# Router scores of the first 1536 tokens computed between the last attention rounds instead of behind them

## The chip, the cores and the metric

One Trainium2 chip, one of its cores. The metric is device time in microseconds (us), the median of several executions; lower is better. Engines are called PE (TensorE), DVE (VectorE), ACT (ScalarE), POOL (GpSimd) and SP (SyncE, which issues most DMAs).

## The reference

Three layers follow each other. Batch 4, 8 heads, 576 positions, head size 64, so 2304 tokens of width 512.

```python
scores = q @ k.T / 8                       # masked: 4 heads local (32 back), 4 heads strided (every 32nd)
attn = exp(scores - max) / (sum + 1e-9)
x = (attn @ v)  -> [2304, 512]
skip_score = x @ w_skip                    # > 0: the token goes to an expert, else it is passed on
logits = x[do] @ w_gate                    # 8 experts, the largest logit chooses; gate = its softmax value
x[do] += gate * (relu(x[do] @ w1[e]) @ w2[e])
h = x @ w_in;  g = h>=1: h, h<=-1: 0, else (h+1)^2/4
out = g @ w_out
```

What the change touches is the product of x with `w_gate` and `w_skip` together, nine scores for a token.

## The kernel before, in words

**Attention.** It is cut into 20 steps (`STEPS`, five for each of four batches of 576 tokens). A round of PE (L915 to L918, and the unrolled epilogue at L919 to L925) does for three different steps: `turn` (L868, four 128x128 transposes of the probabilities), `scores` (not in the epilogue) and `values` (L876, many small products on 64x64 tiles of the array). DVE takes maxima and sums, POOL scales the probabilities (L447, semaphore `normed`), ACT does the exponentials, copies the turned probabilities out of PSUM (L528, `turn_copied`) and places the result of `values` in the tile XT (L537, L543, L546, `x_placed`). `values(n)` waits for `turn_copied` of its own step and for `x_placed` of the step before, since all steps use the same PSUM pair `out_b` (banks 4 and 5).

The epilogue serves steps 16 to 19: the loop is over `range(STEPS, STEPS + LAST)` with LAST = 4, so s = 20, 21, 22, 23, and a pass does `turn(s - 3)` and `values(s - 4)`. The first three passes have both, the fourth has `values(19)` alone. Between them stand products with zeros that nobody reads (`busy`, L829, bf16, 128x512, into bank 3): 1, 0, 1, 0 of them after the four turns (`BUSY_TURNED`) and 4, 0, 2, 2 after the four values (`BUSY_VALUED`).

**Scores of the router.** Behind the epilogue PE waits for all 20 steps to be placed and runs `logits` (L934). The weights `wgs` are 32 columns wide (9 used), and four strips of 512 tokens are put on four 32-column tiles of the array (`out[32*j : 32*(j+1)]`), accumulated over the four 128-blocks of the width (c). That is 16 products of 512 tokens in bank 4, then 8 of 128 tokens (two strips) in bank 5. The scores stand with the score down the partitions, so they are copied (`lgT`, DVE L687, ACT L558), transposed back (PE L946, L949) and copied to `lg` with the token down the partitions (DVE L689, L691).

**Routing.** DVE does a chain of small operations on `lg` (L692 to L740), in which each waits for the one before. Three other engines take part. ACT computes the exponentials (L564), but only behind its copy of row tile 4 (`EXP_AT`). PE computes the ranks of the tokens (L956, L957) behind its row tile 7 (`RANKS_BEHIND`). DVE then ends in `slot_of` (L717), the place of each token in the order sorted by expert.

**Rows.** Meanwhile PE turns XT to rows, 18 tiles of 128 tokens (`rows`, L928, four transposes each, into banks 0 to 3 in turn), and ACT copies each out (L561). PE does `rows(0)` and `rows(1)` ahead of the transposes of the scores and the other 16 behind them.

**Scatter.** When `slot_of` is there, POOL issues 18 indirect DMAs (L456), one after the other, which write the rows to DRAM in sorted order. PE waits for the last eight of them (`late_out`) and runs more products that nobody reads meanwhile (L965). SP waits for all 18, then loads the first windows back (`xfirst`, L368), PE turns them (L970), and the experts begin (L1000, L1010). Behind the experts come the two dense products (L1043, L1056), which take more than half of the time.

**Queues.** SP issues the first three expert weight loads of 2 MB each (L352, L355) when `values(19)` is done.

Of the kernel before, what the change touches and what calls it, by code (L numbers as in the profile page):

```python
# [9 lines left out]
F32 = mybir.dt.float32  # L10
# [8 lines left out]
P = 128  # L19
B, H, S, HD = 4, 8, 576, 64  # L20
STRIDE = 32
PHASE = S // STRIDE
D, E, FE, FF = H * HD, 8, 1024, 2048
N = B * S
NT = N // P
DC, FEC, FFC = D // P, FE // P, FF // P
# [45 lines left out]
TB = len(TILES_OF)  # L72
STEPS = B * TB
# [2 lines left out]
RANKS_BEHIND = 7  # L76
START_BUSY = 10
BUSY_FIRST = [6, 6, 0, 0, 0]
BUSY_TURNED = [1, 0, 1, 0]
BUSY_VALUED = [4, 0, 2, 2]  # L80
BUSY_FROM, BUSY_SCATTER, BUSY_LOAD = 10, 4, 8
SLOTS = TB
LAG, LAST = 3, 4
# [13 lines left out]
REST = N - FULL * G  # L97
EXTRA = (N - 1) // WIN
LGW = 32


MASKS = 5
# [8 lines left out]
def program(nc, qT, kT, vl, vs, wg, w1, w2, win, wout, cst, out):  # L111
    with ExitStack() as ctx:
        def sem(name):
            return ctx.enter_context(nc.semaphore(name))
# [4 lines left out]
        def at(name, shape, dt, offset=None):  # L119
            size = int(np.prod(shape[1:])) * (2 if dt == BF16 else 4)  # L120
            size = (size + 63) // 64 * 64
            where = top[0] if offset is None else offset
            t = nc.alloc_sbuf_tensor_at(name, list(shape), dt, offset=where)
            if offset is None:
                top[0] += size
            return t, where, where + size


        XT, _, _ = at("XT", [P, DC, XCOLS], F32)

        WE1, w_at, w_end = at("WE1", [P, 2, DC, FE], F32)
        WE2, _, w_end = at("WE2", [P, 2, FEC, D], F32)
        o = w_at
        q_loc, _, o = at("q_loc", [P, 2, S], F32, o)
        k_loc, _, o = at("k_loc", [P, 2, S], F32, o)
        v_loc, _, o = at("v_loc", [P, LOC, 4 * HD], F32, o)
        q_str, _, o = at("q_str", [P, 2, S], F32, o)
        k_str, _, o = at("k_str", [P, 2, S], F32, o)
        v_str, _, o = at("v_str", [P, STRIP_PAIRS - 1, 4 * HD], F32, o)
        v_rest, _, o = at("v_rest", [P, 3, 4 * HD], F32, o)  # L140
        assert o <= w_end
        WOH, _, o = at("WOH", [P, FFC, D], F32R, w_at)
        WOL, _, o = at("WOL", [P, FFC, D], F32R, o)
        assert o <= w_end

        WIH, r_at, _ = at("WIH", [P, DC, FF], F32R)
        WIL, _, r_end = at("WIL", [P, DC, FF], F32R)
        xrow, _, o = at("xrow", [P, NT, ROW], F32, r_at)
        prob, p_at, o = at("prob", [P, SLOTS, 512], F32, o)
        probT, _, o = at("probT", [P, 3, 512], F32, o)  # L150
        assert o <= r_end
        gateT, _, o = at("gateT", [E, XCOLS], F32, p_at)
        assert o <= r_end

        hid, h_at, _ = at("hid", [P, 2, FEC, WIN], F32)
        xw, _, _ = at("xw", [P, BUFS, DC, WIN], F32)
        gb, _, _ = at("gb", [P, 2, WIN], F32)
# [13 lines left out]
        cl, _, _ = at("cl", [P, G], F32)  # L171
# [19 lines left out]

        NE9, NE8 = NT * (E + 1), NT * E
        o = h_at
        lgT, _, o = at("lgT", [P, 512 + P], F32, o)
        lg, _, o = at("lg", [P, NT, E + 1], F32, o)
        top8, _, o = at("top8", [P, NT], F32, o)
        dif, _, o = at("dif", [P, NT, E], F32, o)
# [27 lines left out]
        idle_b = bank[3]  # L225
        probT_b = bank[2]
        row_b, logit_b, gate_b = bank[0:4], bank[6], bank[7]
        lgT_b, lgT_rest_b = bank[4], bank[5]
        hid_b, y_b = bank[0:2], bank[2:6]
        first_b, sort_b = bank[2:6], bank[2:6]  # L230
        h2_b, fin_b = bank[6:8], bank[0:4]
# [14 lines left out]
        summed, guarded, inverted, normed, turned, turn_copied = sem("summed"), sem("guarded"), sem("inverted"), sem("normed"), sem("turned"), sem("turn_copied")  # L246
        pv_done, x_placed = sem("pv_done"), sem("x_placed")
        rows_ready, rows_copied, logits_ready = sem("rows_ready"), sem("rows_copied"), sem("logits_ready")
        lgT_ready, lgT_main, lgT_rest, lg_main = sem("lgT_ready"), sem("lgT_main"), sem("lgT_rest"), sem("lg_main")
        route, dif_ready, oh_ready, exp_ready, ranks_ready, slots_ready, aux_ready, starts_ready = sem("route"), sem("dif_ready"), sem("oh_ready"), sem("exp_ready"), sem("ranks_ready"), sem("slots_ready"), sem("aux_ready"), sem("starts_ready")  # L250
        scattered, pads_out = sem("scattered"), sem("pads_out")
        late_out = [sem(f"late_out{t}") for t in range(BUSY_FROM, NT)]
# [267 lines left out]
        def _(act):  # L520
# [33 lines left out]
                if 0 <= s - LAST:  # L554
                    place(s - LAST)

            act.wait_ge(lgT_ready, 2)
            act.copy(lgT[0:2 * LGW, 512:512 + P], lgT_rest_b[0:2 * LGW, 0:P]).then_inc(lgT_rest, 1)  # L558
            for t in range(NT):
                act.wait_ge(rows_ready, t + 1)  # L560
                act.copy(xrow[:, t, 0:D], row_b[t % 4][:, :]).then_inc(rows_copied, 1)  # L561
# [77 lines left out]
        def _(dve):  # L639
# [34 lines left out]
            def link(ins):  # L674
                ins.then_inc(route, 1)
                done[0] += 1
                dve.wait_ge(route, done[0])
# [6 lines left out]
            dve.tensor_copy(xrow[:, :, AUX + E], con[:, C_TOK:C_TOK + NT]).then_inc(aux_ready, 1)  # L684
            link(dve.memset(ones[:, :], 1.0))
            dve.wait_ge(lgT_ready, 1)
            dve.tensor_copy(lgT[:, 0:512], lgT_b[:, :]).then_inc(lgT_main, 1)  # L687
            dve.wait_ge(logits_ready, 2)
            dve.tensor_copy(lg[:, 0:16, :].rearrange("p (j q) e -> p q j e", q=4), logit_b[:, :].rearrange("p (q j e) -> p q j e", q=4, j=4)[:, :, :, 0:E + 1]).then_inc(lg_main, 1)  # L689
            dve.wait_ge(lg_main, 1)  # L690
            link(dve.tensor_copy(lg[:, 16:NT, :], gate_b[:, 0:2 * LGW].rearrange("p (j e) -> p j e", j=2)[:, :, 0:E + 1]))  # L691
            link(dve.tensor_reduce(top8[:, :], lg[:, :, 0:E], AX_X, ALU.max))  # L692
            link(dve.tensor_tensor(dif[:, :, :], lg[:, :, 0:E], tiles(top8[:, :]), ALU.subtract))
            dve.sem_inc(dif_ready, 1)
# [131 lines left out]
        def _(pe):  # L826


            def busy(products, out=None):  # L829

                for _ in range(products):
                    pe.matmul(idle_b[:, :] if out is None else out, warm[:, 0:P], warm[:, :], start=True, stop=True)
# [66 lines left out]
            def round_of(scoring, turning, valuing):  # L899

                if turning:
                    turn(*turning[:2])
                scores(*scoring)
                if valuing:
                    values(*valuing)
# [7 lines left out]
            with pe.Fori(0, LOOPS) as b:  # L913
                for k in range(FIRST, FIRST + TB):
                    round_of(*((TB * b + k - lag, (k - lag) % TB, b + (k - lag) // TB) for lag in (0, LAG, LAST)))  # L915
            for s in range(STEPS, STEPS + LAST):
                if step(s - LAG):
                    turn(*step(s - LAG)[:2])  # L918
                busy(BUSY_TURNED[s - STEPS])  # L919
                values(*step(s - LAST))  # L920
                busy(BUSY_VALUED[s - STEPS])


            pe.wait_ge(wg_in, 16)
            pe.wait_ge(con_in, 16)  # L925
            pe.wait_ge(x_placed, STEPS)
            def rows(t):
# [3 lines left out]
                    last = pe.transpose(row_b[t % 4][:, P * c:P * (c + 1)], XT[:, c, P * t:P * (t + 1)], ident)  # L931
                last.then_inc(rows_ready, 1)

            def logits(out, width, first, groups):  # L934
                for c in range(DC):
                    for j in range(groups):
                        last = pe.matmul(out[LGW * j:LGW * (j + 1), 0:width], wgs[:, c, :], XT[:, c, first + width * j:first + width * (j + 1)], start=(c == 0), stop=(c == DC - 1), skip_group_check=True)  # L937
                last.then_inc(lgT_ready, 1)

            logits(lgT_b, 512, 0, 4)  # L940
            logits(lgT_rest_b, P, 2048, 2)
            for t in range(2):
                rows(t)
            pe.wait_ge(lgT_main, 1)
            for q in range(4):
                last = pe.transpose(logit_b[:, P * q:P * (q + 1)], lgT[:, P * q:P * (q + 1)], ident)  # L946
            last.then_inc(logits_ready, 1)
            pe.wait_ge(lgT_rest, 1)
            pe.transpose(gate_b[:, 0:2 * LGW], lgT[0:2 * LGW, 512:512 + P], ident[0:2 * LGW, 0:2 * LGW]).then_inc(logits_ready, 1)  # L949
            for t in range(2, NT):  # L950
                rows(t)
                if t == RANKS_BEHIND:
# [185 lines left out]
```

## Time and profile before

| what | us |
|---|---|
| runs of the kernel | 687.99, 693.40, 691.78; median 691.78 |
| the profiled execution, its own time | 691.78 |
| its span, first to last instruction | 690.0 |
| attention, up to the end of the last `values` | 0 to 80.1 |
| router scores, routing, scatter, first windows | 80.1 to 125.6 |
| experts | 125.6 to 283.7 |
| dense products and output | 283.7 to 690 |

The profiled execution's own time is 1.8 us more than its span. Over the whole span PE is busy 94%, DVE 46%, ACT 27%, POOL 18%, and the mean granted clock of TensorE is 0.974 of full speed. Each of the stages in the table begins with what the one before it leaves.

### The profile page before, as it was taken

What the parts mean: (1) busy time and instruction counts of PE and PEld (TensorE: products, weight loads), DVE (VectorE), ACT (ScalarE), POOL (GpSimd) and SP (SyncE); (2) the same over time, 40 slices, a digit from 0 to 9 for tenths busy, and PEclk for the clock granted to TensorE, in tenths of its full rate; (3) what the DMA queues carried; (4) which work ended last, traced back from release to release, by engine and by line L of the source; (5) the groups of instructions that cost most, each with busy time, mean ns of one, the idle gap of its engine ahead of it and who ended that gap; (6) DMA issues with size and microseconds to landing.
All of it is one profiled execution on the core that took longest, in us unless ns stands there. A gap on an engine that the chain in (4) does not pass through costs nothing.

```text
span 690.0 us, 12493 instructions
## 1 busy us (share of the span) xinstructions
PE 648.0 (94%) x5190; PEld 553.9 (80%) x5195; DVE 314.8 (46%) x570; ACT 187.9 (27%) x361; POOL 126.9 (18%) x135
## 2 busy tenths in 40 slices
PE   7888856899999999899999999999999999999995
PEld 3767642899999999788888888888888888888994
DVE  4766250141122121675446644456545565545652
ACT  2545450141111111222224222233222332223331
POOL 1323145002222224882000200002000020000201
PEclk9999986999999999999999999999999999999998
DMA  8676495964777775330000100001000010000100
GB/s 285 225 257 226 166 359 198 352 228 167 262 253 255 257 258 178 94 106 16 1 0 1 62 0 1 0 1 61 0 0 0 0 61 0 0 0 0 62 1 30
DMA packets 39477, 76.34 MB, mean 111 GB/s; under 512 B 3079, under 2 KB 17844, under 8 KB 38916
## 3 DMA queue, kind: packets, MB, share of 16 engines
q1 hardware_dynamic: 36556, 66.26, 28.1%
q0 software_dynamic: 2880, 9.52, 3.6%
q8 instruction: 28, 0.46, 0.3%
q14 instruction: 13, 0.11, 0.1%
HBM read 65.83 MB, written 9.94 MB: 110 GB/s over the span
## 4 chain that ended last, share of the span: by engine, by line
PE 81%; DMA 9%; POOL 3%; DVE 2%; issue 1%; SPq 1%; ACT 1%; DVEq 0%
PE pair L1043 28%; PE pair L1056 16%; PE bank L1056 13%; PE pair L1000 9%; DMA WE<-w 4%; PE out_pair L1010 4%; PE bank L1010 4%; DMA k_str<-kT 2%; POOL x_sorted L456 2%; PE out_pair L895 2%; PE pair L853 2%; DMA k_loc<-kT 1%; PE bank L873 1%; DMA xfirst<-x_sorted 1%; PE out_pair L937 1%
## 5 line engine op out<-in xcount | busy, mean ns | idle before, releaser
L1043 PE MATMUL pair<-yh,WIH 128*128 128x512 f32 (+1 forms) x320 | 116.7, 371 | 0.2 <-ACT yh L596 0.2
L1043 PE MATMUL pair<-yh,WIL 128*128 128x512 f32 (+1 forms) x320 | 116.5, 370 | 0.0
L620 ACT ACTIVATE cl<-cl,half 128x512 f32<-128x512 f32 (+1 forms) x80 | 54.5, 681 | 186.9 <-DVE cl L808 185.5
L816 DVE TENSOR_TENSOR gl<-gr,gh 128x512 fp32r<-128x512 f32 (+1 forms) x80 | 54.1, 677 | 73.6 <-ACT gh L629 72.5
L808 DVE TENSOR_SCALAR cl<-pair 128x512 f32<-128x512 f32 (+1 forms) x80 | 50.9, 637 | 73.0 <-PE pair L1043 73.0
L515 POOL DMA_INDIRECT out<-XT,tok x18 | 18.6, 1031 | 351.6 <-DVE XT L796 347.6
L1043 PE MATMUL pair<-yl,WIH 128*128 128x512 f32 (+1 forms) x320 | 79.7, 369 | 1.7 <-DVE yl L787 1.7
L1000 PE MATMUL pair<-xw,WE 128*128 128x168 f32 x512 | 76.2, 311 | 0.2
L1000 PEld LDWEIGHTS pair<-xw,WE 128*128 128x128 f32 x512 | 74.8, 193 | 0.8 <-DMA WE<-w 0.7
L1043 PEld LDWEIGHTS pair<-yh,WIH 128*128 128x128 f32 x320 | 60.7, 190 | 11.3 <-ACT yh L596 0.6
L629 ACT CAST gh<-gr 128x512 fp32r<-128x512 f32 (+1 forms) x80 | 46.3, 579 | 86.0 <-PE bank L1056 61.0
L1043 PEld LDWEIGHTS pair<-yh,WIL 128*128 128x128 f32 x320 | 60.9, 190 | 10.7
L1043 PEld LDWEIGHTS pair<-yl,WIH 128*128 128x128 f32 x320 | 57.0, 189 | 12.7 <-DVE yl L787 2.8
L814 DVE TENSOR_TENSOR gr<-gr,cl 128x512 f32<-128x512 f32 (+1 forms) x80 | 52.7, 659 | 22.3 <-ACT cl L620 22.0
L1056 PE MATMUL pair<-WOH,gh 128*128 128x512 f32 x160 | 62.5, 391 | 0.0
L1056 PE MATMUL pair<-WOL,gh 128*128 128x512 f32 x160 | 62.4, 390 | 0.0
L1056 PE MATMUL pair<-WOH,gl 128*128 128x512 f32 x160 | 62.3, 389 | 0.0
L811 DVE TENSOR_SCALAR gr<-pair 128x512 f32<-128x512 f32 (+1 forms) x80 | 50.1, 627 | 0.0
L577 ACT ACTIVATE hid<-pair 128x168 f32<-128x168 f32 x64 | 19.9, 310 | 110.2 <-PE pair L1000 110.2
L1056 PE MATMUL bank<-WOH,gh 128*128 128x512 f32 x128 | 49.8, 389 | 0.0
L1056 PE MATMUL bank<-WOL,gh 128*128 128x512 f32 x128 | 49.8, 389 | 0.0
L1056 PE MATMUL bank<-WOH,gl 128*128 128x512 f32 x128 | 49.8, 389 | 0.0
(144 smaller groups left out, 814.4 us busy)
## 6 DMA issues: line engine op xcount, KB each, us to landing
WE<-w SPq DMA_DIRECT2D x16, 2048.0 KB, 12.3
xrow<-x_sorted SPq DMA_DIRECT2D x6, 781.5 KB, 9.1
v_loc<-vl SPq DMA_DIRECT2D x4, 1024.0 KB, 7.8
raw_in<-win SPq DMA_DIRECT2D x16, 256.0 KB, 9.5
raw_out<-wout SPq DMA_DIRECT2D x16, 256.0 KB, 2.6
q_loc<-qT SPq DMA_DIRECT2D x4, 576.0 KB, 6.1
k_loc<-kT SPq DMA_DIRECT2D x4, 576.0 KB, 8.1
v_str<-vs SPq DMA_DIRECT2D x8, 256.0 KB, 4.2
```

Source lines behind the costliest of these rows:

```text
L515: pool.indirect_dma_start(out, bass.IndirectOffsetOnAxis(tok[:, GT * g + t:GT * g + t + 1], 0), rows_of(g, t), None).then_inc(out_done if ...
L577: act.activation(hid[:, par, f, :], hid_b[f % 2][:, 0:WIN], ACT.Relu).then_inc(h_done, 1)
L620: act.activation(cl[:, 0:n], cl[:, 0:n], ACT.Square, bias=half[:, :], scale=0.5).then_inc(squared, 1)
L629: act.copy(gh[:, f % 2, 0:n], gr[:, 0:n]).then_inc(g_high, 1)
L808: dve.tensor_scalar(cl[:, 0:n], h2_b[f % 2][:, 0:n], -1.0, 1.0, ALU.max, ALU.min).then_inc(clamped, 1)
L811: dve.tensor_scalar(gr[:, 0:n], h2_b[f % 2][:, 0:n], 1.0, -1.0, ALU.max, ALU.add).then_inc(over, 1)
L814: dve.tensor_tensor(gr[:, 0:n], gr[:, 0:n], cl[:, 0:n], ALU.add).then_inc(g_ready, 1)
L816: dve.tensor_tensor(gl[:, f % 2, 0:n], gr[:, 0:n], gh[:, f % 2, 0:n].bitcast(F32), ALU.subtract).then_inc(g_low, 1)
L1000: last = pe.matmul(hid_b[f % 2][:, 0:WIN], WE1[:, par, c, P * f:P * (f + 1)], xw[:, buf, c, :], start=(c == 0), stop=(c == DC - 1))
L1010: last = pe.matmul(y_b[c][:, 0:WIN], WE2[:, par, f, P * c:P * (c + 1)], hid[:, par, f, :], start=(f == 0), stop=(f == FEC - 1))
L1043: last = pe.matmul(h2_b[f % 2][:, 0:tokens], w[:, c, P * f:P * (f + 1)], x[:, c, 0:tokens], start=(k == 0), stop=(k == 3 * DC - 1))
L1056: last = pe.matmul(fin_b[t][:, :], x[:, f % 2, P * t:P * (t + 1)], w[:, f, :], start=(f == 0 and k == 0), stop=(f == FFC - 1 and k == 2))
```

## The change

The scores are cut anew: three strips of 512 tokens (tokens 0 to 1535, `EARLY`) and three strips of 256 tokens (tokens 1536 to 2303, `LATE`).

```diff
-BUSY_TURNED = [1, 0, 1, 0]
-BUSY_VALUED = [4, 0, 2, 2]
+STRIPS, EARLY, LATE = 3, 512, 256
+LG_EARLY = STRIPS * EARLY // P
-        lgT_b, lgT_rest_b = bank[4], bank[5]
+        lgT_b, lgT_rest_b = bank[3], bank[4]
...
-            act.wait_ge(lgT_ready, 2)
-            act.copy(lgT[0:2 * LGW, 512:512 + P], lgT_rest_b[0:2 * LGW, 0:P]).then_inc(lgT_rest, 1)
...
             dve.wait_ge(lgT_ready, 1)
-            dve.tensor_copy(lgT[:, 0:512], lgT_b[:, :]).then_inc(lgT_main, 1)
-            dve.wait_ge(logits_ready, 2)
-            dve.tensor_copy(lg[:, 0:16, :].rearrange("p (j q) e -> p q j e", q=4), logit_b[:, :].rearrange("p (q j e) -> p q j e", q=4, j=4)[:, :, :, 0:E + 1]).then_inc(lg_main, 1)
-            dve.wait_ge(lg_main, 1)
-            link(dve.tensor_copy(lg[:, 16:NT, :], gate_b[:, 0:2 * LGW].rearrange("p (j e) -> p j e", j=2)[:, :, 0:E + 1]))
+            dve.tensor_copy(lgT[0:STRIPS * LGW, 0:EARLY], lgT_b[0:STRIPS * LGW, :]).then_inc(lgT_main, 1)
+            dve.wait_ge(lgT_ready, 2)
+            dve.tensor_copy(lgT[0:STRIPS * LGW, EARLY:EARLY + LATE], lgT_rest_b[0:STRIPS * LGW, 0:LATE]).then_inc(lgT_rest, 1)
+            for k, (first, last, turned_b) in enumerate(((0, LG_EARLY, logit_b), (LG_EARLY, NT, gate_b))):
+                q = (last - first) // STRIPS
+                dve.wait_ge(logits_ready, k + 1)
+                link(dve.tensor_copy(lg[:, first:last, :].rearrange("p (j q) e -> p q j e", q=q),
+                                     turned_b[:, 0:(last - first) * LGW].rearrange("p (q j e) -> p q j e", q=q, j=STRIPS)[:, :, :, 0:E + 1]))
...
+            def logits(out, width, first, c):
+                for j in range(STRIPS):
+                    last = pe.matmul(out[LGW * j:LGW * (j + 1), 0:width], wgs[:, c, :], XT[:, c, first + width * j:first + width * (j + 1)], start=(c == 0), stop=(c == DC - 1), skip_group_check=True)
+                if c == DC - 1:
+                    last.then_inc(lgT_ready, 1)
             for s in range(STEPS, STEPS + LAST):
                 if step(s - LAG):
                     turn(*step(s - LAG)[:2])
-                busy(BUSY_TURNED[s - STEPS])
+                if s == STEPS + 2:
+                    logits(lgT_b, EARLY, 0, 1)
                 values(*step(s - LAST))
-                busy(BUSY_VALUED[s - STEPS])
-            pe.wait_ge(wg_in, 16)
+                if s == STEPS:
+                    pe.wait_ge(wg_in, 16)
+                    pe.wait_ge(x_placed, TB * (B - 1))
+                    logits(lgT_b, EARLY, 0, 0)
+                elif s >= STEPS + 2:
+                    logits(lgT_b, EARLY, 0, s - STEPS)
             pe.wait_ge(con_in, 16)
             pe.wait_ge(x_placed, STEPS)
...
-            logits(lgT_b, 512, 0, 4)
-            logits(lgT_rest_b, P, 2048, 2)
+            for c in range(DC):
+                logits(lgT_rest_b, LATE, STRIPS * EARLY, c)
+            for k, (at_, width, turned_b, signal) in enumerate(((0, EARLY, logit_b, lgT_main), (EARLY, LATE, gate_b, lgT_rest))):
+                pe.wait_ge(signal, 1)
+                for q in range(width // P):
+                    last = pe.transpose(turned_b[:, STRIPS * LGW * q:STRIPS * LGW * (q + 1)], lgT[0:STRIPS * LGW, at_ + P * q:at_ + P * (q + 1)], ident[0:STRIPS * LGW, 0:STRIPS * LGW])
+                last.then_inc(logits_ready, 1)
             for t in range(2):
                 rows(t)
-            pe.wait_ge(lgT_main, 1)
-            for q in range(4):
-                last = pe.transpose(logit_b[:, P * q:P * (q + 1)], lgT[:, P * q:P * (q + 1)], ident)
-            last.then_inc(logits_ready, 1)
-            pe.wait_ge(lgT_rest, 1)
-            pe.transpose(gate_b[:, 0:2 * LGW], lgT[0:2 * LGW, 512:512 + P], ident[0:2 * LGW, 0:2 * LGW]).then_inc(logits_ready, 1)
```

So a slice, three products of 512 tokens for one c, stands behind `values(16)` (c = 0), ahead of `values(18)` (c = 1), behind `values(18)` (c = 2) and behind `values(19)` (c = 3). All `busy` products of the epilogue go. The transposes of the scores stand ahead of `rows(0)` and `rows(1)`, and the copy of the second part of `lgT` goes from ACT to DVE.

## Rows read from the trace of the kernel before

**Rows 1.** The profile page, its part 4: the chain that ended last, by engine.
```profile
PE 81%; DMA 9%; POOL 3%; DVE 2%; issue 1%; SPq 1%; ACT 1%; DVEq 0%
```

**Rows 2.** Timeline of PE, 66 to 104 us; columns: start us, length us, engine, line, operation
```profile
71.57 0.73 PE L895 MATMUL out_pair<-probT,v_str 64*64 64x54 f32 x32 [0.44 <-ACT XT L537]
72.23 1.04 PE L832 MATMUL bank<-warm 128*128 128x512 bf16 x4
73.46 0.66 PE L873 MATMUL bank<-con,prob 128*128 128x128 f32 x4 [0.19 <-POOL prob L447]
74.04 1.05 PE L895 MATMUL out_pair<-probT,v_rest 64*64 64x54 f32 x48
75.02 0.65 PE L873 MATMUL bank<-con,prob 128*128 128x128 f32 x4
76.09 1.74 PE L895 MATMUL out_pair<-probT,v_loc 64*64 64x32 f32 x64 [0.42 <-ACT XT L543]
...
78.59 1.46 PE L895 MATMUL out_pair<-probT,v_loc 64*64 64x32 f32 x64 [0.23 <-ACT XT L546]
...
80.83 4.50 PE L937 MATMUL out_pair<-XT,wgs 128*32 128x512 f32 x48 [0.24 <-ACT XT L546]
85.26 1.09 PE L931 MATMUL pair<-con,XT 128*128 128x128 f32 x8
86.19 0.60 PE L946 MATMUL pair<-con,lgT 128*128 128x128 f32 x4
...
90.04 0.54 PE L956 MATMUL pair<-oh,con 128*128 128x162 f32 x2 [0.28 <-DVEq L702]
```

**Rows 3.** Timeline of DVE, 70 to 128 us
```profile
84.59 0.69 DVE L687 COPY lgT<-out_pair 128x512 f32<-128x512 f32 x1 [10.72 <-PE out_pair L937]
...
87.58 0.30 DVE L692 TENSOR_REDUCE top<-lg 128x18 f32<-128x144 f32 x1
...
90.08 0.30 DVE L705 TENSOR_REDUCE gate<-ex 128x18 f32<-128x144 f32 x1 [0.15 <-DVE oh L701]
...
91.15 0.32 DVE L711 COPY tot<-pair 128x162 f32<-128x162 f32 x1
...
93.59 0.18 DVE L717 CAST slot_of<-posf 128x18 uint32<-128x18 f32 x1
```

**Rows 4.** Timeline of POOL, 66 to 128 us: first and last of the 18 scatters
```profile
94.06 1.14 POOL L456 DMA_INDIRECT x_sorted<-xrow,slot_of  x1 [13.64 <-ACT xrow L561]
...
115.74 0.96 POOL L456 DMA_INDIRECT x_sorted<-xrow,slot_of  x1 [0.30 <-issue]
```

**Rows 5.** Timeline of PE's weight loads (PEld), 66 to 128 us
```profile
81.25 0.15 PEld L937 LDWEIGHTS out_pair<-XT,wgs 128*32 128x32 f32 x4 [0.28 <-issue]
81.68 0.16 PEld L937 LDWEIGHTS out_pair<-XT,wgs 128*32 128x32 f32 x4 [0.27 <-issue]
...
84.26 0.80 PEld L937 LDWEIGHTS out_pair<-XT,wgs 128*32 128x32 f32 x14 [0.28 <-issue]
```

**Rows 6.** Timeline of ACT, 66 to 128 us
```profile
80.09 0.58 ACT L546 COPY XT<-out_pair 128x512 f32<-128x512 f32 x1 [1.65 <-PE out_pair L895]
...
85.95 1.07 ACT L561 COPY xrow<-pair 128x512 f32<-128x512 f32 x2 [0.33 <-PE pair L931]
...
89.05 0.35 ACT L564 ACTIVATE ex<-dif 128x144 f32<-128x144 f32 x1
...
95.15 1.18 ACT L561 COPY xrow<-pair 128x512 f32<-128x512 f32 x2
```

**Rows 7.** Timeline of PE, 105 to 190 us: products of the first two experts
```profile
125.61 11.01 PE L1000 MATMUL pair<-xw,WE 128*128 128x168 f32 x64
...
146.27 9.29 PE L1000 MATMUL pair<-xw,WE 128*128 128x168 f32 x64
```

**Rows 8.** Busy time by 2 us: PE, PEld, DVE, ACT, POOL, PEclk, DMA share, GB/s
```profile
122.00:124.00 2.00, 0.32 (x3) 0.32 (x4) 0.00 (x0) 0.00 (x0) 0.00 (x0) 1.00 0.73 188
...
126.00:128.00 2.00, 2.00 (x8) 2.00 (x8) 0.02 (x1) 0.01 (x1) 0.00 (x0) 0.50 1.00 382
```

More of the change, by code:

```diff
@@ L99 @@
 LGW = 32
+STRIPS, EARLY, LATE = 3, 512, 256
+LG_EARLY = STRIPS * EARLY // P
+assert STRIPS * (EARLY + LATE) == N and STRIPS * EARLY <= (B - 1) * S
 MASKS = 5
@@ L193, in program @@
         o = h_at
-        lgT, _, o = at("lgT", [P, 512 + P], F32, o)
+        lgT, _, o = at("lgT", [P, EARLY + LATE], F32, o)
         lg, _, o = at("lg", [P, NT, E + 1], F32, o)
@@ L248, in program @@
         rows_ready, rows_copied, logits_ready = sem("rows_ready"), sem("rows_copied"), sem("logits_ready")
-        lgT_ready, lgT_main, lgT_rest, lg_main = sem("lgT_ready"), sem("lgT_main"), sem("lgT_rest"), sem("lg_main")
+        lgT_ready, lgT_main, lgT_rest = sem("lgT_ready"), sem("lgT_main"), sem("lgT_rest")
         route, dif_ready, oh_ready, exp_ready, ranks_ready, slots_ready, aux_ready, starts_ready = sem("route"), sem("dif_ready"), sem("oh_ready"), sem("exp_ready"), sem("ranks_ready"), sem("slots_ready"), sem("aux_ready"), sem("starts_ready")
@@ L932, in rows @@
                 last.then_inc(rows_ready, 1)
[L934 to L938, printed above, removed]
-            logits(lgT_b, 512, 0, 4)
-            logits(lgT_rest_b, P, 2048, 2)
+            for c in range(DC):
[5 more added lines that the diff above has]
+                last.then_inc(logits_ready, 1)
             for t in range(2):
                 rows(t)
-            pe.wait_ge(lgT_main, 1)
-            for q in range(4):
-                last = pe.transpose(logit_b[:, P * q:P * (q + 1)], lgT[:, P * q:P * (q + 1)], ident)
-            last.then_inc(logits_ready, 1)
-            pe.wait_ge(lgT_rest, 1)
-            pe.transpose(gate_b[:, 0:2 * LGW], lgT[0:2 * LGW, 512:512 + P], ident[0:2 * LGW, 0:2 * LGW]).then_inc(logits_ready, 1)
             for t in range(2, NT):
```

## The prediction, made before the changed kernel was run

> **What bounds the kernel now.** I read the chain that ended last first. PE holds 81% of it [rows 1], so over the whole span the kernel is bound by products. That says nothing of the stretch that the change touches, so I went on to the timelines from 70 to 128 us, one engine at a time.
>
> There the chain goes in single file: last attention steps, router scores, transposes, DVE's routing chain, scatter, experts. The reader should see three things. First, the last `values` start on an ACT copy: at 76.09 and 78.59 PE had been idle for 0.42 and 0.23 us and was released by XT L543 and L546 [rows 2], although products that nobody reads stand in the gaps. Second, behind the placement of step 19 (ACT, 80.09 plus 0.58 [rows 6]) PE needs 4.50 us for the scores, and the routing chain reads `lg` at 87.58 only [rows 2, 3]. Third, POOL starts its 18 scatters at 94.06, 0.3 us after `slot_of` (93.59 plus 0.18), and issues them at one per (115.74 - 94.06) / 17 = 1.275 us, whatever the others do [rows 3, 4]. The rows are copied faster than that (18 from 85.95 to 96.33 us [rows 6]), so the scatter begins with `slot_of`, and the experts begin a fixed time behind the scatter. What moves `slot_of` moves the end.
>
> **The change part by part.**
>
> *What a slice costs.* The four 32-column tiles work beside each other: four weight loads come per 0.43 us (81.25 to 81.68 [rows 5]), and each 512-token product has two such records, so one c of four strips takes 2 x 0.43 = 0.86 us. Three strips on three tiles should take the same 0.86 us, since each tile has its own strip to stream. Bounds: 0.64 us, if the time goes by the number of products (6 x 0.107), and 6 x 0.43 = 2.6 us, if the strips ran one after another. I take 0.86, since the rows show exactly this form with one tile more. Between array layouts (128x128 turns, 64x64 values) the rows leave little: four turns at 73.46, at 0.11 us each, are followed by values at 74.04, so 0.14 us at most. I add 0.10 us ahead of each slice and 0.14 behind.
>
> The Trainium skill (TensorEngine Tiling (Array Packing), Key Properties) says that changing the tiling mode drains TensorE. That speaks against slicing, because each slice brings layout changes that the scores in one piece do not have. By the rows' 0.14 us the drain is already in my sum; the page gives no figure of its own.
>
> *c = 0, behind `values(16)`.* It takes the place of four products (72.23, 1.04 us) ahead of the turn at 73.46, which waits for POOL (0.19 us idle [rows 2]). Values end at about 72.25; 0.10 + 0.86 + 0.14 gives 73.35. It costs 0. The cover is POOL's scaling, with 0.1 us left. The waits on `wg_in` and on 15 placed steps are long met: values of step 16 themselves waited for 16.
>
> *c = 1, ahead of `values(18)`.* The turns at 75.02 issue until 75.46 (4 x 0.11). With the slice values(18) start at 75.46 + 1.10 = 76.56 in place of 76.09: **+0.47 us**. Queued behind it on PE is all that follows, and ACT's placement waits for it.
>
> *c = 2, behind `values(18)`.* From the start of values(18) to that of values(19) it is 78.59 - 76.09 = 2.50 us now, of which about 1.6 are the values' own issue. With the slice it is 1.6 + 1.10 = 2.7: **+0.2 us**. So values(19) start at 79.26, its placement at 80.76, ending at 81.34.
>
> *c = 3 and the late strips.* Values(19) issue until 80.66; the slice runs to 81.62, behind the placement, so the wait for step 20 placed costs nothing. The late part is 4 c of 2 records of 256 tokens: 8 x 0.214 = 1.71 us, to 83.33. Before, the scores ended at 80.83 + 4.50 = 85.33. The 128-token part took 0.80 us for 14 of 16 loads [rows 5]; 24 loads at that rate take 1.4 us and stay under 1.71.
>
> *The way to `lg`.* DVE's copy of the first part (0.69 us [rows 3]) runs beside the late strips. Its four transposes take 0.44 us, to 83.87. The copy of the second part, 256 wide, begins at 83.5; between the 162-wide copy (0.32) and the 512-wide one (0.69 [rows 3]) I take 0.42, so 83.95; two transposes end at 84.35; the second copy to `lg` ends at 84.70. (Before, `rows(0)` and `rows(1)` stood ahead: 86.19 - 85.26 = 0.93 us [rows 2].) The routing chain begins at 84.70 in place of 87.58: **-2.88 us**.
>
> *What is late next.* The chain does not keep all of that. Rows now begin at 84.25, 1.0 us earlier than 85.26, and not 2.9. ACT's first copy goes from 85.95 to about 84.94; five copies at 0.53 us (1.07 for two [rows 6]) and the exponential of 0.35 us end at 87.75 or so (between 87.5 and 88.1). DVE, with everything else shifted, would want it at 90.08 - 2.88 = 87.20. So the reduction L705 starts near 87.80: 0.6 us are given back, and the shift is **-2.28 us**. The ranks: eight row tiles at 0.435 us from 84.25 end at 87.73, and 0.82 us more for the ranks is 88.55, against DVE's need at 91.15 - 2.28 = 88.87 [rows 2, 3]. This wait has 0.3 us left.
>
> *Behind it.* `slot_of` comes 2.3 us earlier, so the scatter starts at 91.8. The expert weights are asked for by the end of values(19), 0.67 us later than before, and are needed at 125.6 less 2.3, so this costs 0. They share the DMA engines with the early scatters; only the last scatters are waited for, and those are issued at POOL's own pace. All later DMAs hang on events that move along. The copy moved from ACT to DVE has 0.42 us, already in the sum.
>
> The sum: the profiled execution took 691.78 us, span 690.0 and 1.8 around it, and is the median of the runs. 691.78 - 2.28 = 689.5.
>
> **The rivals.**
>
> *The clock's low spells shift.* In the first expert the granted clock stands at 0.50 of full speed (1.2 in place of 2.4 GHz) at 126 to 128 us, after PE had done only 0.32 us of work at 122 to 124 [rows 8]. That expert's 64 products take 11.01 us where the next one's take 9.29: a spell costs 1.7 us [rows 7]. The spell comes late after the idle time, so another moment of arrival may avoid it or add one: 687.8 or 691.2. For it: the spread of the runs, 5.4 us. Against: PE's pattern ahead of the experts is the same, only earlier. The lost filling products are not a way to a new spell, I think: their time is taken by slices.
>
> *ACT keeps up.* If exponential and ranks do not hold DVE, all 2.88 us come through: 688.9. It needs copies at 0.45 us, faster than any row.
>
> *ACT's row copies bound the scatter.* The row of the first scatter names the ACT copy as releaser [rows 4]. Then only the 1.0 us of the rows count: 690.8. Against: the first scatter needs one copied tile, and that was there at 86.5.
>
> *Slower: strips in single file.* If three strips in a slice do not overlap because both records of one product must finish ahead of the next product, a slice takes up to 2.6 us. With x for a slice, c = 1, 2, 3 and the late part (two slices' worth) put 5 x on the path, and the gain of 2.28 is gone at x = 0.86 + 2.28 / 5 = 1.3 us. At 2.6 it is 5 x 1.7 more, and c = 0 overruns its cover by 1.5: 691.8 - 2.3 + 8.5 + 1.5 = 699.5. Against: four strips in the same order overlap fully now [rows 5].
>
> *It does not do what it says* (nothing moves, because the wait for POOL or ACT in the last rounds sets all): excluded by the 4.50 us, which have no such wait in them.
>
> **How the numbers follow.** Forecast 689.5 with chance 0.60; a low spell less 0.12; one more 0.12; all 2.88 us 0.06; bound by row copies 0.05; strips in single file 0.03; something outside this stretch by more than 1%, 0.02. A measurement of this kernel can tell about 1% (7 us) from no change. All cases but the last two lie within it: same 0.95, faster 0.02, slower 0.03. The range takes in the clock cases at 687.8 and 691.2 and 1 us more each side for the spread of the runs, whose median moves by about that: 686.8 to 692.3.
>
> **What would show it right or wrong.** Right: 24 + 24 records of 512 and 256 tokens in place of 32 and 16; values(18) and (19) start 0.47 and 0.67 us later; reduction L692 at 84.7; DVE idle for about 0.6 us ahead of the reduction of the gates, released by ACT; first scatter near 91.8, last near 113.5; experts from 123.3; equal lengths behind. Wrong: a slice of more than 1.1 us; the turn behind c = 0 later than 73.5; a new fall of the clock between 72 and 90 us; a wait of DVE for the ranks; an expert stage that starts earlier but lasts longer.

## The result, and the profile after

The changed kernel took 685.86 us (median of 20 runs, 681.68 to 689.11), the kernel before 689.29 (20 runs, 686.29 to 694.03): ratio 0.994, 95% interval 0.9922 to 0.9958, that is 4.1 us less (2.9 to 5.4). The ratio is one of means (685.86 and 689.84); the medians lie 3.4 us apart. The forecast was 689.5 with a range from 686.8, so the time lies 0.9 us below the range. Two later copies of the changed kernel gave 0.9965 (0.9937 to 0.9993) and 0.9955 (0.9928 to 0.9982).

The profiled execution took 683.28 us, its span is 681.5, 8.5 less than before. Most of that does not lie where the change acts. I cut both spans at the turns of step 18 (the second last four turns of probabilities), the first scatter, the first expert's first product, and the first turn of sorted rows behind that expert:

| stretch, us | before | after | difference |
|---|---|---|---|
| start to turns of step 18 (of the change only the slice behind `values(16)` lies here) | 73.46 | 70.83 | -2.63 |
| turns of step 18 to first scatter (the change) | 20.60 | 17.86 | -2.74 |
| first scatter to first expert | 31.55 | 30.28 | -1.27 |
| first expert's 64 products | 10.84 | 9.23 | -1.61 |
| the rest of the span | 553.55 | 553.30 | -0.25 |

Timeline of PE of the changed kernel, 70 to 100 us, which answers to [rows 2] (columns as there; L876 are the turns, L898 the values, L921 the slices and late strips, L945 the rows):

```profile
69.59 1.06 PE L921 MATMUL bank<-XT,wgs 128*32 128x512 f32 x6
70.83 0.66 PE L876 MATMUL bank<-con,prob 128*128 128x128 f32 x4 [0.18 <-POOL prob L449]
...
72.39 0.66 PE L876 MATMUL bank<-con,prob 128*128 128x128 f32 x4
72.98 1.06 PE L921 MATMUL bank<-XT,wgs 128*32 128x512 f32 x6
73.97 1.46 PE L898 MATMUL out_pair<-probT,v_loc 64*64 64x32 f32 x64
75.35 1.06 PE L921 MATMUL bank<-XT,wgs 128*32 128x512 f32 x6
76.34 1.45 PE L898 MATMUL out_pair<-probT,v_loc 64*64 64x32 f32 x64
77.73 1.06 PE L921 MATMUL bank<-XT,wgs 128*32 128x512 f32 x6
78.61 1.90 PE L921 MATMUL out_pair<-XT,wgs 128*32 128x256 f32 x24
80.44 0.99 PE L953 MATMUL pair<-con,lgT 96*128 96x96 f32 x6
81.27 1.04 PE L945 MATMUL pair<-con,XT 128*128 128x128 f32 x8
```

The turns at 70.83 still wait for POOL, so the slice ahead of them was free. From 72.39 on PE has no idle time left between these rows, where [rows 2] has 0.42, 0.23 and 0.24 us. (Of the 0.42 us a part was filled: the trace of before has records of six of the ten filling products. The trace of e12, a run of the same attention code that is described below, has all ten, and 0.21 us idle there.) A slice is 72.98 to 73.97, 0.99 us. Two times 0.43 us are the products, as in [rows 5], and 0.13 us are left behind them; ahead of the slice it is 0.15 us (72.39 to 72.98, less 4 x 0.11 for the turns). The Trainium skill (TensorEngine Tiling (Array Packing), Key Properties) says that changing the tiling mode drains TensorE. The trace agrees in so far as these 0.13 and 0.15 us lie at the changes of layout; no run here shows that a drain is what fills them.

Timeline of DVE of the changed kernel, 70 to 128 us, for [rows 3]:

```profile
81.78 0.30 DVE L695 TENSOR_REDUCE top<-lg 128x18 f32<-128x144 f32 x1
...
84.70 0.30 DVE L708 TENSOR_REDUCE gate<-ex 128x18 f32<-128x144 f32 x1 [0.57 <-ACT ex L564]
...
88.21 0.18 DVE L720 CAST slot_of<-posf 128x18 uint32<-128x18 f32 x1
```

Timeline of POOL, the same stretch, first and last scatter, for [rows 4]:

```profile
88.69 1.14 POOL L458 DMA_INDIRECT x_sorted<-xrow,slot_of  x1 [10.52 <-ACT xrow L561]
...
110.42 0.96 POOL L458 DMA_INDIRECT x_sorted<-xrow,slot_of  x1 [0.30 <-issue]
```

The reduction of the largest score is L695 here and L692 in the kernel before; below I call it L692 in both. The new wait is in the second line of DVE: it stands for 0.57 us until the exponential is done, where before it waited only 0.15 us behind its own work [rows 3].

Behind the scatter, for [rows 7], timeline of PE, 98 to 190 us:

```profile
116.55 0.97 PE L977 MATMUL bank<-con,xfirst 128*128 128x128 f32 x8
118.02 1.03 PE L977 MATMUL out_pair<-con,xfirst 128*128 128x128 f32 x8 [0.49 <-DMA xfirst<-x_sorted]
118.97 9.39 PE L1007 MATMUL pair<-xw,WE 128*128 128x168 f32 x64
```

The idle time ahead of the first expert is short here, and it runs at full clock. Whether that is the change's was the question for the experiments.

### The profile page after: what moved, and what is told of

Read it like the earlier page. It is cut to its first block, busy times and chain, and to the rows that moved or that the text cites. A ratio compares the mean times of both kernels' runs of the same rounds, so it can differ in the third digit from the quotient of the medians.

```text
span 681.5 us, 12481 instructions
## 1 busy us (share of the span) xinstructions
PE 641.6 (94%) x5185; PEld 548.7 (81%) x5186; DVE 316.6 (46%) x571; ACT 188.0 (28%) x360; POOL 126.7 (19%) x135
## 4 chain that ended last, share of the span: by engine, by line
PE 84%; DMA 6%; POOL 3%; DVE 2%; issue 1%; ACT 1%; SPq 1%; DVEq 0%
PE pair L1050 29%; PE pair L1063 16%; PE bank L1063 13%; PE pair L1007 10%; PE out_pair L1017 5%; PE bank L1017 5%; DMA k_loc<-kT 3%; POOL x_sorted L458 2%; DMA WE<-w 2%; PE out_pair L898 2%; PE pair L856 2%; ACT xrow L561 1%; PE bank L876 1%; DVE yl L790 1%; PE bank L991 1%
## 5 line engine op out<-in xcount | busy, mean ns | idle before, releaser
L1007 PE MATMUL pair<-xw,WE 128*128 128x168 f32 x512 | 74.5, 306 | 0.2 <-DMA WE<-w 0.2
L1007 PEld LDWEIGHTS pair<-xw,WE 128*128 128x128 f32 x512 | 73.2, 190 | 0.5 <-DMA WE<-w 0.5
## 6 DMA issues: line engine op xcount, KB each, us to landing
xrow<-x_sorted SPq DMA_DIRECT2D x6, 781.5 KB, 10.2
```

Of the source, the lines that this page charges most:

```text
L1007: last = pe.matmul(hid_b[f % 2][:, 0:WIN], WE1[:, par, c, P * f:P * (f + 1)], xw[:, buf, c, :], start=(c == 0), stop=(c == DC - 1))
```

## The experiments

All stretches are those of the table, in us of one profiled execution; median and ratio are those of 12 runs (six for e9). "xf" is last scatter to the first turns of xfirst.

| run | edit | start to turns of 18 | to first scatter | scatter to expert | xf | first expert | rest | median us | ratio (95%) |
|---|---|---|---|---|---|---|---|---|---|
| e0 | before | 72.66 | 20.35 | 31.44 | 7.84 | 10.90 | 550.85 | 688.62 | 0.9996 (0.997 to 1.0022) |
| e2 | new cut, not moved | 73.68 | 20.83 | 31.47 | 7.56 | 10.46 | 551.86 | 688.96 | 0.9996 (0.9961 to 1.0031) |
| e3 | turns of scores first | 70.24 | 19.87 | 33.07 | 8.16 | 11.00 | 553.12 | 688.42 | 1.0009 (0.998 to 1.0037) |
| e6 | before, no fill | 75.94 | 23.14 | 30.91 | 6.13 | 9.23 | 552.98 | 688.76 | 0.9992 (0.9968 to 1.0016) |
| e10 | before, no fill | 72.89 | 23.17 | 31.38 | 5.81 | 10.16 | 552.90 | 692.33, one run | |
| e12 | before, padded | 70.84 | 20.69 | 30.94 | 6.17 | 10.90 | 550.93 | 688.48 | 0.9999 (0.9971 to 1.0028) |
| e1 | after | 74.73 | 17.86 | 31.05 | 6.17 | 10.90 | 552.96 | 685.79 | 0.9965 (0.9937 to 0.9993) |
| e14 | after | 74.46 | 17.85 | 31.17 | 5.82 | 10.90 | 553.12 | 686.53 | 0.9955 (0.9928 to 0.9982) |
| e7 | after, padded | 71.32 | 17.85 | 31.84 | 7.44 | 11.54 | 553.55 | 687.34 | 0.9957 (0.9935 to 0.9979) |
| e13 | after, padded | 73.29 | 17.86 | 30.99 | 6.68 | 10.66 | 553.00 | 685.78 | 0.9953 (0.9928 to 0.9979) |
| e8 | slice c = 0 late | 73.35 | 20.25 | 30.39 | 5.91 | 9.23 | 553.28 | 687.53 | 0.9965 (0.9945 to 0.9985) |
| e4 | exponential early | 73.31 | 17.60 | 31.05 | 6.22 | 10.47 | 553.37 | 687.61, one run | |
| e5 | and ranks early | 74.97 | 17.44 | 30.89 | 6.02 | 10.90 | 551.00 | 685.18 | 0.9949 (0.9923 to 0.9975) |
| e11 | as e5 | 71.03 | 17.43 | 30.90 | 5.88 | 10.90 | 550.34 | 684.62 | 0.9947 (0.9927 to 0.9966) |
| e9 | e5 and four fills | 70.36 | 17.45 | 31.45 | 5.96 | 9.23 | 553.01 | 683.10 | 0.992 (0.9895 to 0.9946) |
| e15 | e9, padded | 70.85 | 17.43 | 31.20 | 6.25 | 9.22 | 549.80 | 683.75 | 0.9926 (0.9898 to 0.9953) |

**The changed kernel again (e1), and the kernel before again (e0).**

> The changed kernel once more, for a second profile. Stretches are measured from the start of the second last pair of turns that wait for POOL, the turns of step 18 (before 73.46 us, after 70.83 us). Theory A (the change gives a fixed 2.75 us between the turns of step 18 and the first scatter; the remaining difference of the two profiled spans is spread from run to run): turns of step 18 to first scatter 17.9 us again, but start to the turns of step 18 anywhere in 70 to 74 us, first scatter to first expert 30.2 to 31.6, first expert's 64 products 9.3 or 11.0. Theory B (the change itself also makes the transfers and the clock behind the scatter better): first scatter to first expert 30.3 again and first expert 9.3 again. Time 0.994 to 0.996 of before.

> The kernel before once more, for a second profile. Theory C: behind the scatter the kernels differ because an instruction fetch (one packet of the queue of kind instruction) falls beside the loads of the first windows (xfirst) in the kernel before, at 120 us, and not in the changed one, whose PE program is nine products shorter up to there. Then here again: a fetch between the first xfirst load and the first turns of xfirst; last scatter to the first of these turns 7.5 to 8.2 us (after: 6.0 to 6.2), first scatter to first expert 31.5 or more. Theory A (spread from run to run): values like those of the changed kernel, 6.1 and 30.3 to 31.1, are as likely.

The stretch of the change repeats to 0.01 us (17.86), the others do not: e1 starts its turns 3.9 us later than the first profile and has a first expert of 10.90 us, for the same program. So theory A (spread from run to run) holds for the attention and the first expert, whose 2.63 and 1.61 us are spread. The granted clock goes with the spread. In the five profiles in which it stood at 1.00 up to the turns of step 18 (after, e3, e7, e9, e12) these come at 70.2 to 71.3 us, in the thirteen others, with a mean of 0.93 to 0.98, at 70.9 to 75.9. The first expert takes 9.2 us in the five profiles in which the clock stands at 1.00 all through it (after, e6, e8, e9, e15) and 10.2 to 11.5 in the thirteen in which it is at 0.50 for a part. And the rest of the span is 552.9 to 553.6 us in the twelve profiles in which the clock falls to 0.50 between 281 and 296 us, and 549.8 to 551.9 in the six in which it does not (e0, e2, e5, e11, e12, e15). Kernels with and without the change are on either side each time but one (no kernel with the filling products of before has the 9.2), so the spread is not tied to the change as far as is shown. e1's ratio, 0.9965, is just above the expected 0.994 to 0.996. xf repeats in each kernel (6.13, 6.17 against 7.94, 7.84), which A did not say.

**The new cut without the move (e2).**

```diff
+                busy(BUSY_TURNED[s - STEPS])
                 values(*step(s - LAST))
+                busy(BUSY_VALUED[s - STEPS])
-                if s == STEPS + 2:
-                    logits(lgT_b, EARLY, 0, 1)
-                if s == STEPS:
...
-                    pe.wait_ge(x_placed, TB * (B - 1))
-                    logits(lgT_b, EARLY, 0, 0)
-                elif s >= STEPS + 2:
-                    logits(lgT_b, EARLY, 0, s - STEPS)
...
+            for c in range(DC):
+                logits(lgT_b, EARLY, 0, c)
```

> Three strips of 512 and three of 256 tokens and the turns of the scores ahead of the rows, but all of it behind the attention, with the filling products back in the epilogue. If the move between the last rounds is what brings the gain: turns of step 18 to first scatter 20.8 us (before 20.6, after 17.9), time within 0.1% of before. Rival (the new cut and the new order of the turns bring it): below 19.5 us.

20.83 us, and a ratio of 0.9996: the cut and the new order of the turns alone bring nothing (before and e0 have 20.60 and 20.35). The move, with the filling products that it replaces, brings 20.83 - 17.86 = 2.97.

**Only the turns of the scores ahead of the rows (e3).**

> The kernel before with one edit: the turns of the scores ahead of rows 0 and 1. The reduction L692 comes 0.9 us earlier against the turns of step 18. If the exponential behind ACT's copy of row tile 4 holds DVE, 0.4 us of it are given back: turns of step 18 to first scatter 20.1 us. If it does not: 19.7.

Against e0, whose values take the same 1.46 us, the reduction L692 comes 0.79 us earlier and the scatter 0.48. DVE waits 0.47 us for the exponential. So 0.3 us, two fifths of what the order of the turns gives, are lost to the same wait. As time the 0.48 us do not show (ratio 1.0009).

**The exponential and the ranks (e5, e4).** `EXP_AT = 4` to 1, and in e5 `RANKS_BEHIND = 7` to 6.

> The changed kernel with the exponential behind ACT's copy 1 instead of 4 and the ranks behind row tile 6 instead of 7. If the wait of 0.57 us ahead of the reduction of the gates is the exponential's place in ACT's queue: the wait goes, turns of step 18 to first scatter 17.3 us (after 17.9), time about 0.9992 of after. If something else holds DVE there, 17.9.

> The changed kernel with only the exponential moved, behind copy 1. The wait of 0.57 us for it goes; then the ranks, behind row tile 7, come 0.2 to 0.3 us too late for DVE: turns of step 18 to first scatter 17.6 to 17.7 us, between 17.86 (changed kernel) and 17.44 (both moved).

Timeline of DVE, e4, 82 to 94 us:

```profile
86.76 0.30 DVE L708 TENSOR_REDUCE gate<-ex 128x18 f32<-128x144 f32 x1 [0.15 <-DVE oh L704]
...
87.60 0.31 DVE L711 TENSOR_TENSOR xrow<-oh,gate 128x144 f32<-128x144 f32 x1
87.99 0.33 DVE L714 COPY tot<-pair 128x162 f32<-128x162 f32 x1
```

The wait for the exponential is gone. L714 begins 0.39 us after L711 where it is 0.22 in the changed kernel (85.55 to 85.77): the ranks are late next, by 0.17 us. With both moved the stretch is 17.44, 0.42 less (expected 17.3). Both steps were as expected in the trace; the time of e5 and e11 (0.9949 and 0.9947) can't be told from that of the changed kernel, 0.994 to 0.9965.

**The filling products and the slice behind step 16 (e6, e10, e8).** e6 and e10 set `BUSY_TURNED` and `BUSY_VALUED` of the kernel before to zero. e8 is the changed kernel with the slices c = 0 ahead of values(18), 1 behind them, 2 and 3 behind values(19), and none behind step 16.

> The kernel before without the ten products that nobody reads in the epilogue of the attention, nothing else. Turns of step 18 to first scatter as before, 20.3 to 20.6 us. Theory C: the PE program is ten products shorter, so the fetch moves into the first expert, and last scatter to first turns of xfirst falls to 6.1 us, first scatter to first expert to 30.3 to 31.1; time about 0.9985 of before. Theory A: 7.5 to 8.2 and 31.5 as in the kernel before. If the filling products hold the clock up, the granted clock falls between 72 and 90 us and the stretch gets over 1 us longer.

> The kernel before without its ten filling products, a second profile. Last scatter to first turns of xfirst 6.1 us again, whatever the clock does. The fall of the clock at 81 to 87 us that its first profile showed may come again (turns of step 18 to first scatter 23.1 us) or not (20.3): it depends on when the idle gaps fall.

> The changed kernel with one slice fewer behind values of step 16 and one more behind values of step 19. If the slice behind step 16 is free and one behind step 19 costs its whole 0.86 us: turns of step 18 to the reduction L692 11.8 us (after 10.95), to first scatter 18.7 (after 17.9). If slices cost nothing because something else ends last: 17.9.

Both profiles without fill have the same 2.8 us more (23.14, 23.17 against e0's 20.35). Busy time by 2 us of e6 (columns: PE, PEld, DVE, ACT, POOL, granted clock, DMA share, GB/s):

```profile
78.00:80.00 2.00, 1.58 (x66) 1.37 (x64) 0.00 (x0) 0.87 (x4) 0.00 (x0) 1.00 0.00 0
80.00:82.00 2.00, 1.22 (x40) 1.22 (x40) 0.00 (x0) 0.58 (x1) 0.00 (x0) 0.73 0.03 8
82.00:84.00 2.00, 1.22 (x39) 1.12 (x36) 0.00 (x0) 0.59 (x1) 0.23 (x1) 0.50 0.00 0
```

Timeline of PE of e6, 70 to 98 us:

```profile
75.94 0.66 PE L873 MATMUL bank<-con,prob 128*128 128x128 f32 x4 [1.17 <-POOL prob L447]
...
80.81 2.40 PE L895 MATMUL out_pair<-probT,v_loc 64*64 64x32 f32 x64 [0.78 <-ACT XT L546]
83.99 6.34 PE L937 MATMUL out_pair<-XT,wgs 128*32 128x512 f32 x48 [0.78 <-ACT XT L546]
```

With the gaps left open (1.17 us ahead of the turns of step 18, 0.42 ahead of values(18), 0.78 ahead of values(19) and of the scores), the clock goes from 2.4 to 1.2 GHz, and the scores take 6.34 us where they took 4.50 [rows 2]. Which of the gaps it takes is not shown. Nor does the loss show in the runs: e6 has 0.9992 (0.9968 to 1.0016) of before, so at most 1.1 us more, and its profiled execution, 693.96 us, was one of its slowest. The fall may be a matter of single executions, or be made up for behind the scatter. e8 missed its expectation, 20.25 in place of 18.7, by a fall of the clock too. Timeline of PE of e8, 70 to 98 us:

```profile
73.35 0.63 PE L876 MATMUL bank<-con,prob 128*128 128x128 f32 x4 [1.37 <-POOL prob L449]
...
76.17 1.93 PE L921 MATMUL bank<-XT,wgs 128*32 128x512 f32 x6
```

Busy time of e8 by 2 us:

```profile
72.00:74.00 2.00, 0.65 (x6) 0.51 (x8) 1.50 (x5) 0.94 (x3) 1.60 (x2) 1.00 0.04 12
74.00:76.00 2.00, 2.00 (x52) 1.79 (x52) 0.00 (x0) 1.35 (x4) 0.48 (x1) 0.64 0.00 0
76.00:78.00 2.00, 2.00 (x8) 0.20 (x6) 0.00 (x0) 0.63 (x2) 0.00 (x0) 0.51 0.00 0
78.00:80.00 2.00, 2.00 (x73) 1.50 (x70) 0.00 (x0) 0.47 (x1) 0.00 (x0) 1.00 0.04 8
```

PE stands idle for 1.37 us ahead of the turns, the clock falls, and values(18) begin 1.54 us later (4.68 after the turns of step 18, against 3.14). L692 comes at 13.35 after them: 10.95, plus 1.54, plus 0.86 for the slice that now lies on the path. So the slice behind step 16 is free, and in this profile its absence also let the clock fall. The time does not show these 2.4 us: e8 has 687.53 us, and e7, the changed kernel with padding measured beside it, 687.34. The Trainium skill (TensorE: Matmul & The Clock Gate, What's actually happening) says that the throttled state is the default and activity releases it. The trace agrees: the clock is at 0.51 at 76 to 78 us, behind the idle time, and back at 1.00 at 78 to 80, with PE busy from 74 us on.

**Where the instruction fetch falls (e7, e12, e13, e14).** The trace has two queues of kind instruction, which I read as the engines' instruction fetches. One, q14, puts a packet of 8 KB some 2.9 to 4.0 us behind the first xfirst load in every profile. The other, q8, with packets of 16 KB, is the one that moves, and "the fetch" is its packet. In the kernel before, it comes at 120.8 us, between the first xfirst load (118.65) and the first turns of xfirst (123.68); in the changed kernel, whose PE program is nine products shorter up to there, it comes at 121.6 us, in the first expert (118.97 to 128.2). e7 and e13 put nine products into PE's idle time behind the last row tile of the changed kernel, e12 puts 36 there in the kernel before:

```diff
             pe.wait_ge(slots_ready, 1)
+            for _ in range(9):
+                pe.matmul(bank[0][:, :], ident_b[:, :], mask_b[:, 0, :].unsqueeze(1).to_broadcast([P, 8, KEYS]), start=True, stop=True)
```

> The changed kernel with nine products that nobody reads put on PE behind its last row tile, where it then sits idle for 15 us: the PE program is as long again as before up to the first windows. Turns of step 18 to first scatter 17.9 us as in the changed kernel. Theory C: a fetch beside the loads of xfirst again, last scatter to first turns of xfirst 7.5 to 8.2 us, first scatter to first expert 31.5. Theory A: 6.1 and 30.3 to 31.1.

> The kernel before with 36 products that nobody reads behind PE's last row tile, where PE then sits idle: they lengthen the PE program, so that the instruction fetch comes earlier, ahead of the loads of xfirst. Turns of step 18 to first scatter 20.3 to 20.6 us as before. Theory C: last scatter to first turns of xfirst falls from 7.8 to 6.0 us and first scatter to first expert from 31.5 to 30.3 to 31.1; time 0.9985 of before. Rival (what helps is the changed scores, not where the fetch falls): 7.8 and 31.5.

> The changed kernel with nine products of padding once more, beside the changed kernel itself. Theory C: last scatter to first turns of xfirst 7.4 to 8.2 us, first scatter to first expert 31.4 or more, time about 1 us over the changed kernel. Rival: no difference.

> The changed kernel a third time, as the partner of the padded one. Turns of step 18 to first scatter 17.86 us, last scatter to first turns of xfirst 6.0 to 6.2, first scatter to first expert 30.3 to 31.1; time 0.9945 to 0.995 of before if 2.5 to 2.75 us of the new order and about 1 us of the fetch add up.

The fetch lies between first load and first turns in before, e0, e2, e3, e7, e13: xf is 7.4 to 8.2 us in five of the six, 6.68 in e13. In the twelve others it lies elsewhere, and xf is 5.8 to 6.25. e12 moves it by padding alone (to 108.6 us) and xf falls from 7.84 to 6.17; e6 moves it the other way (to 132.4 us) with the same result. So when the first window is ready goes with the place of the fetch. It is worth less behind that, since PE also needs the second window: scatter to first expert has a mean of 31.73 us over those six and 30.97 over the twelve. A third of this 0.8 us is e3 alone (33.07); the medians are 31.51 and 31.0. e13 missed its expectation: 6.68 us and 30.99, which is no more than its partner e14 has (31.17). As time, nothing of it is shown: e12 measures 0.9999 of before where 0.9985 was expected, and e13, expected 1 us over the changed kernel, has 685.78 us beside e14's 686.53. Theory C (the fetch delays the windows) stands in the trace, with e13 as half an exception, and not in the metric.

**The fastest version (e9, e11, e15).** e9 is e5 with four fills between the turns of the two xfirst tiles; e15 adds 36 products of padding.

```diff
+                if par == 0:
+                    for _ in range(4):
+                        pe.matmul(bank[0][:, :], ident_b[:, :], mask_b[:, 0, :].unsqueeze(1).to_broadcast([P, 8, KEYS]), start=True, stop=True)
```

> The changed kernel with the exponential behind copy 1, the ranks behind row tile 6, and four more products that nobody reads between the turns of the first and of the second xfirst, where PE sits idle for 0.5 to 1.2 us. Turns of step 18 to first scatter 17.4 us. If that idle time is what lets the clock fall in the first expert: first expert 9.2 us always, granted clock 1.00 there, time 0.5 to 1 us below the kernel with the early exponential alone. If not: 10.9 in a share of executions as before, no difference in time. The fetch stays behind the turns of xfirst.

> The changed kernel with the exponential behind copy 1 and the ranks behind row tile 6, once more beside the filled one on the same chip: turns of step 18 to first scatter 17.4 us, last scatter to first turns of xfirst 6.0 to 6.2 us, time 0.995 of before.

> The filled kernel with early exponential, whose fetch fell at 118.5 us beside the second xfirst load, with 36 products of padding in PE's idle time. Theory C: no fetch between the first xfirst load and the first expert, first scatter to first expert 30.3 to 31.1 in place of 31.45, first expert 9.2, time 0.991 of before or a little under.

Timeline of PE of e5, 116 to 130 us:

```profile
120.16 1.02 PE L977 MATMUL bank<-con,xfirst 128*128 128x128 f32 x8
122.34 1.03 PE L977 MATMUL out_pair<-con,xfirst 128*128 128x128 f32 x8 [1.17 <-DMA xfirst<-x_sorted]
```

Timeline of PE of e9, 114 to 130 us:

```profile
116.46 1.04 PE L981 MATMUL pair<-mask_b,ident_b 128*128 128x512 bf16 x4
118.31 1.03 PE L977 MATMUL out_pair<-con,xfirst 128*128 128x128 f32 x8 [0.81 <-DMA xfirst<-x_sorted]
119.26 9.39 PE L1010 MATMUL pair<-xw,WE 128*128 128x168 f32 x64
```

With the fill both profiles have a first expert of 9.2 us; e5 and e11 have 10.90. Three of the sixteen profiles without this fill have 9.2 us too (after, e6, e8), so two profiles do not prove the "always" of the expectation. The medians are 683.10 (six runs) and 683.75 beside 684.62 (e11), 0.992 and 0.9926 of before, the lowest of all. The part of the fill would be 0.9 to 1.5 us, expected were 0.5 to 1; the intervals of e9 and e11 overlap, so neither its size nor that it helps is settled. In e9 the fill moved the fetch to 118.5 us. That is 0.2 us behind the start of the turns of the second window (118.31), so the fetch did not hold them up, other than the expectation of e15 says; e15 moved it to 107.9 us without a gain in time.

## Why the prediction was right or wrong

**What failed is the base, not the mechanism.** The forecast was "691.78 - 2.28", from the profiled execution, which was also the median of three runs. The kernel's own time is lower: medians of 689.29, 688.19, 689.25, 688.99 and 689.25 in five sets of 17 to 35 runs. The prediction allowed 1 us on each side for the spread of the runs; its base was 2.5 us too high. 689.3 - 2.3 would have been 687.0, still 1.1 us above the measured 685.86: 0.2 to 0.5 of this are the mis-sized term below, the rest is spread. The five stretches show why one execution is a poor base: the attention up to the turns of step 18 spreads over 70.2 to 75.9 us, the first expert over 9.2 to 11.5, the rest over 549.8 to 553.6, each with the granted clock of that stretch.

**Terms.** The slice behind values(16) at 0: right (the wait for POOL is 0.18 us, before 0.19). The clock that its absence cost in the profile of e8 was not foreseen. c = 1 at +0.47: 0.51 (3.14 for 2.63). c = 2 at +0.2 took 1.6 us for the values' own issue, though the same sum has 1.40 for values(19); it is 1.38 (73.97 to 75.35). So values(18) to values(19) is 2.38 us, forecast 2.7. Values(19) at +0.67: 0.63 against e0 (5.51 for 4.88), but 0.38 against the first profile, whose values(18) took 1.74 us where e0's and all of the changed kernel's took 1.46. L692 at -2.88: -2.91 against e0 (10.95 for 13.86), -3.17 against the first profile. The giving back at the exponential, 0.6: a wait of 0.57, of which 0.42 are lost (L692 to the gates 2.92 for 2.50). The first scatter at -2.28: -2.49 against e0 and -2.74 against the first profile; this term was 0.2 to 0.5 us too small, because ACT's copies come at 0.48 us and not 0.53, and the rows began earlier than I put them (10.44 us behind the turns of step 18, forecast 10.79). The 0.53 was a misreading: 1.07 us is the length of a row of two copies [rows 6], and the trace of before has the row behind such a one 0.96 us after it. Timeline of ACT of the kernel before, 66 to 128 us:

```profile
87.61 1.07 ACT L561 COPY xrow<-bank 128x512 f32<-128x512 f32 x2 [0.59 <-PE bank L931]
88.57 0.61 ACT L561 COPY xrow<-pair 128x512 f32<-128x512 f32 x1
```

**Behind the scatter.** "Behind it: this costs 0" was right in time as far as the runs tell. In the trace the stretch from first scatter to first expert was 1.3 us shorter in the first pair of profiles and 0.3 to 0.4 in the later ones (31.05 and 31.17 against e0's 31.44); the instruction fetch, which the prediction did not have, goes with it. The first result, 4.1 us, contains some luck: over its 44 runs in three sets the changed kernel has a mean of 685.97 us, over its 142 in five sets the kernel before has 689.08 (688.95 without the first set). The 3.0 to 3.1 us between them are the 2.5 to 2.7 of the scatter and a rest of 0.3 to 0.6, which is within the spread: single executions of one kernel have a standard deviation of about 2 us.

**Rivals.** Strips in single file: a slice took 0.99 us, not 2.6, so it fell. ACT's copies as bound of the scatter: fell, the scatter follows `slot_of` by 0.3 us again, although the profile names the copy. ACT keeps up: fell, e5 had to move it. The clock's spells: the first expert ran at full clock in the profile of after and not in e1 and e14, so this differs between executions of one kernel and moved single profiles by 1.7 us; that the change shifts how often it happens is not shown.

## What to carry to other kernels

Work moved into the gaps of a chain leaves the path, and it fills the gaps, which matters where the clock would otherwise fall: profiles with some or all of these gaps open had the clock at half behind them (e6, e10, e8), though their run times did not show the loss. When filling products go, put real ones in the same gaps, and look at the granted clock there. When a chain gets shorter, look at every engine that feeds it from its own queue (here the exponential behind the fifth copy, then the ranks behind the eighth row tile) and shift those too. Base a forecast of a fraction of a per cent on many runs, and compare profiles by stretches from an event at which both kernels are still the same.

## What the runs showed of the hardware

Where a 16 KB packet of the instruction queue q8 fell between the first window load and the first turns, these turns came 7.4 to 8.2 us behind the last scatter (6.68 in e13), in place of 5.8 to 6.25. Nine products of padding in the changed kernel brought it there (e7, e13), 36 in the kernel before took it away (e12); no difference in time was measured.

Idle gaps of 0.42 to 1.17 us between short stretches of transposes and 64x64 tiles were enough for the granted clock to fall from 1.00 to 0.50 in both profiles without filling products (e6, e10), and in e8 it fell behind a gap of 1.37 us. With four products in the largest gap and one or two in the others it stood at 1.00 in all five profiles with the attention of before (before, e0, e2, e3, e12). Between array layouts the trace leaves 0.13 to 0.15 us.
